# Shifting every SBUF tensor that TensorE reads to a 2048-byte boundary, with small tensors and a filler in front

## The reference, cut to what matters

```
x = conv7(x, softmax(weight))                  # 8192 tokens x 192
h = x @ w_in;  x = (h * clip(h + 3, 0, 6) / 6) @ w_out
h = x @ w_in2; y = where(h > 0, h, exp(min(h, 0)) - 1) @ w_out2
```

## Time and profile before

| | |
|---|---|
| Time, median of 3 runs | 1156.77 us (1155.81 to 1157.89) |
| The profiled execution: its time | 1156.3 us |
| The profiled execution: span from first to last instruction | 1154.5 us |
| PE busy | 1149.2 us (100% of the span), 9744 matmuls |
| PEld, weight loads | 937.8 us (81%), 9744 loads |
| DVE busy | 903.5 us (78%) |
| ACT busy | 632.5 us (55%) |
| POOL busy | 40.4 us (3%) |
| Mean granted TensorE clock | 1.000 of full speed |

### The profile page before, as it was taken

How to read it: one execution, slowest core, us unless ns; L and a number is a source line. 1 busy time by engine, 2 the same in 40 slices (tenths; PEclk the granted TensorE clock), 3 DMA queues, 4 the chain that set the end, 5 groups by cost and what they waited for, 6 DMA issues and landing times.

```text
span 1154.5 us, 24081 instructions
## 1 busy us (share of the span) xinstructions
PE 1149.2 (100%) x9744; PEld 937.8 (81%) x9744; DVE 903.5 (78%) x963; ACT 632.5 (55%) x684; POOL 40.4 (3%) x36
## 2 busy tenths in 40 slices
PE   9999999999999999999999999999999999999998
PEld 6888888888888888888888888888888888888886
DVE  7897887878778787787877878788787887876766
ACT  6665655546555555555555555555554555546544
POOL 4422000000000000000000000000000000000000
PEclk9999999999999999999999999999999999999999
DMA  4310010100101001010010100101000010000000
GB/s 151 115 38 28 1 33 0 32 0 0 32 0 32 0 0 32 0 32 0 0 32 0 32 0 0 32 0 32 0 18 14 0 32 0 9 5 10 6 2 28
DMA packets 14760, 22.48 MB, mean 19 GB/s; under 512 B 1424, under 2 KB 5520, under 8 KB 14736
## 3 DMA queue, kind: packets, MB, share of 16 engines
q1 hardware_dynamic: 14592, 22.12, 6.1%
q10 hardware_dynamic: 144, 0.01, 0.0%
HBM read 15.83 MB, written 6.29 MB: 19 GB/s over the span
## 4 chain that ended last, share of the span: by engine, by line
PE 99%; DMA 1%; ACT 0%; SPq 0%; DVE 0%; issue 0%; DVEq 0%; ACTq 0%
PE h_ps L674 39%; PE acc_a L688 23%; PE h_ps L681 21%; PE acc_b L697 15%; DMA xnext_b<-x_win 1%; PE acc_a L830 0%; PE h_ps L705 0%; PE acc_a L760 0%; DVE hidden L522 0%; PE acc_a L737 0%; ACT hidden L340 0%; PE acc_a L744 0%; PE acc_a L738 0%; PE acc_b L739 0%; PE acc_b L745 0%; PE acc_b L754 0%
## 5 line engine op out<-in xcount | busy, mean ns | idle before, releaser
L350 ACT CAST g_hi<-hidden 128x1024 fp32r<-128x1024 f32 x255 | 268.0, 1051 | 351.0 <-DVE hidden L527 237.5
L531 DVE TENSOR_TENSOR g_lo<-hidden,g_hi 128x1024 fp32r<-128x1024 f32 x255 | 313.1, 1228 | 127.6 <-ACT g_hi L350 127.6
L688 PE MATMUL acc_a<-g_hi,wout_hi_a 64*128 64x512 f32 x1012 | 398.2, 393 | 0.0
L688 PE MATMUL acc_a<-g_hi,wout_lo_a 64*128 64x512 f32 x1012 | 397.8, 393 | 0.0
L674 PE MATMUL h_ps<-in_lo_a,win_hi_a 64*128 64x512 f32 x1012 | 397.7, 393 | 0.0
L674 PE MATMUL h_ps<-in_hi_a,win_lo_a 64*128 64x512 f32 x1012 | 397.2, 392 | 0.0
L674 PE MATMUL h_ps<-in_hi_a,win_hi_a 64*128 64x512 f32 x1012 | 396.6, 392 | 0.0
L697 PE MATMUL acc_b<-g_hi,wout_b 64*128 64x512 f32 x1012 | 357.2, 393 | 0.0
L688 PE MATMUL acc_a<-g_lo,wout_hi_a 64*128 64x512 f32 x1012 | 317.4, 393 | 0.0
L697 PE MATMUL acc_b<-g_lo,wout_b 64*64 64x512 f32 x1012 | 314.9, 390 | 0.0
L522 DVE SCALAR_TENSOR_TENSOR hidden<-hidden,h_ps 128x1024 f32<-128x1024 f32 x128 | 156.2, 1221 | 77.5 <-ACT hidden L340 77.5
(11 more groups left out here) (109 smaller groups left out, 1207.7 us busy)
## 6 DMA issues: line engine op xcount, KB each, us to landing
xwin_a<-x_win SPq DMA_DIRECT2D x16, 259.0 KB, 2.7
raw_in<-w_in SPq DMA_DIRECT2D x8, 512.0 KB, 4.3
out_t<-out_a SPq DMA_DIRECT2D x16, 256.0 KB, 2.9
xwin_b<-x_win SPq DMA_DIRECT2D x15, 259.0 KB, 2.9
raw_out<-w_out SPq DMA_DIRECT2D x8, 384.0 KB, 3.6
out_t<-out_b SPq DMA_DIRECT2D x16, 128.0 KB, 2.3
xnext_b<-x_win SPq DMA_DIRECT2D x1, 259.0 KB, 6.1
taps<-tap_w ACTq DMA_DIRECT2D x1, 7.0 KB, 2.6
```

The lines of the kernel that those rows point to most:

```text
L350: nc.scalar.copy(g_hi[:, g % PARTS, :], hidden[:, g % 2, :]).then_inc(hi_ready, 1)
L531: nc.vector.tensor_tensor(g_lo[:, g % PARTS, :], hidden[:, g % 2, :], g_hi[:, g % PARTS, :].bitcast(F32), ALU.subtract).then_inc(lo_ready, 1)
L688: return nc.tensor.matmul(acc_a[acc][:, :], w[HALVES[r], g * CPG + c, :], x[HALVES[r], g % PARTS, c * TOK:(c + 1) * TOK], start=g == 0 and ...
```

## The change

The change edits only the order in which SBUF tensors are created, and adds one tensor that nothing uses. `ident`, `taps`, `tap_stat` and `three` are created first, then a `filler` of 1280 bytes a partition; `diag`, `xnext_b`, `xwin_a` and `xwin_b` are created last. On every engine the instructions and their order are the same, row for row, before and after. Only the addresses differ:

| Tensors | Bytes past a multiple of 2048, before | after |
|---|---|---|
| `win_*`, `wout_*`, `raw_in` | 128 | 0 |
| `raw_out0`, `raw_out1` | 128, 1152 | 0, 1024 |
| `conv_a`, `conv_b` | 192 | 0 |
| `in_*`, `hidden`, `g_hi`, `g_lo`, `half_b*`, `sum_b1`, `out_*` | 288 | 0 |
| `diag` | 864 | 0 |
| `xwin_a`, `xwin_b`, `xnext_b` | 128, 160, 320 | 1568, 1600, 1536 |

```
+        ident = sb("ident", [P, 2, DB])
+        taps = sb("taps", [P, 2, TAPS])
+        tap_stat = sb("tap_stat", [P, 2, 3])
+        three = sb("three", [P, 1])
+        sb("filler", [P, 320])
+
         win_hi_a = [sb(f"win_hi_a{m}", [P, FF], F32R) for m in range(2)]
...
         raw_out = [sb(f"raw_out{s}", [P, CPP, D]) for s in range(STAGES)]

-        xwin_a = sb("xwin_a", [DA, WIN])
-        xwin_b = sb("xwin_b", [2 * DB, WIN])
         conv_a = sb("conv_a", [DA, TOK])
         conv_b = sb("conv_b", [2 * DB, TOK])
-        taps = sb("taps", [P, 2, TAPS])
-        tap_stat = sb("tap_stat", [P, 2, 3])
...
-        three = sb("three", [P, 1])
+        diag = sb("diag", [P, TAPS, P])
         xnext_b = sb("xnext_b", [2 * DB, WIN])
-        ident = sb("ident", [P, 2, DB])
-        diag = sb("diag", [P, TAPS, P])
+        xwin_a = sb("xwin_a", [DA, WIN])
+        xwin_b = sb("xwin_b", [2 * DB, WIN])
```

## The result

The changed kernel takes 1131.31 us (1130.99 to 1131.97, 4 runs) against 1156.7 us (1155.81 to 1157.89, 4 runs): a ratio of 0.978, with a 95% interval of 0.976 to 0.980. It is 25 us faster. The time lies in the predicted range, but the forecast called likeliest, no change, is wrong.

A forecast was written before the change was run, and what follows sets the result against it. PE was taken to bound the kernel through the distance between its matmul starts, 233.5 ns a pair. All terms were taken as 0, so the time stays at 1156.5 us, with a range of 1123 to 1168 us (0.84).

The forecast's parts named there:

- no change: Whole kernel: the time does not depend on the addresses and stays at 1156.5 us; chance 0.68.
- What bounds the kernel: Steady stage: only the distance between matmul starts on PE, 233.5 ns a pair, can move the time by much.
- The 20 ns over 213.3 and the suspect: Steady pairs: 233.5 ns against 213.3 at one column a cycle; the reading of the moving operand is suspected.
- Moving operands: Steady pairs: starts go from 288 to 0 past a multiple of 2048; taken as 0, at most 85 us.
- Weight operands: Steady weight chunks: chunks 7 and 9 show the same steps, so taken as 0, at most 12 us back.
- a piece less for each row: Moving rows fetched in 64-byte pieces, 32 in place of 33: 6.7 ns a pair, giving 1124 us; chance 0.09.
- the whole excess goes: All 17.7 ns a steady pair come from the address, 85 us, giving 1071 us; 0.09 for more than one piece less.
- the two reads of TensorE meet: Weight loads and moving stream hinder each other after the change: 6 ns a pair, 29 us, giving 1185 us; chance 0.14.
- The Trainium skill's 16-byte lines: Moving rows: a 2048-byte row from 288 or from 0 touches 128 SBUF lines either way, so 0.
- DVE, ACT and DMAs at 0: Other engines and loads: small changes stay hidden under PE's work, so 0, with 0.6 us either way for DMAs.
- the single stream near the end stays at about 232 ns: Sign of a right prediction: four full-row matmuls near the end, 232.5 ns each before, keep their distance.

The follow-up runs named there:

- all at 32: Changed kernel with a filler 32 bytes longer, so weights and moving operands alike begin 32 bytes past a multiple of 2048: 1131.06 us, ratio 0.978.
- the first two runs: Kernel before with 32 bytes put ahead of `in_hi_a0`: 1153.85 us; changed kernel with a filler 32 bytes longer: 1131.06 us.
- short loads: Most steady matmuls use only 64 of their 128 weight columns: 1141.73 us in the kernel before, 1137.15 us in the changed one.

## Why the prediction was right in its range and wrong in its reason

- **What bounds the kernel**: right. Only the distance between pairs changed, and the time with it.
- **The 20 ns over 213.3 and the suspect**: half right. The convolution's step of 215.8 ns was read as "replacing the weights does not cost 20 ns in itself", and the suspect was the moving read alone. The convolution is no witness for the full rate: by the change its own distance goes from 224 to 0 modulo 256 at the first tap, and its step stays at 215.8 ns. At the full rate it is the moving read and the load together, by their distance, that make 5.3 of the 20 ns.
- **"Moving operands: I take 0, because the only moving start that varies in this trace changes nothing"**: this step failed. It asked for the effect of a start address by itself. That is indeed nothing (all at 32: 1131.1 us); the effect lies in the distance, 25.5 us over 4812 pairs, which the convolution did not test at the full rate.
- **"Weight operands: I take 0"**: this failed too, and for a reason worth seeing. Chunks 7 and 9 in the earlier trace rows begin at different places, but all chunks are multiples of 512 bytes apart, so their distances to the moving rows are the same modulo 256. The comparison could not have shown the effect.
- **The rival "a piece less for each row"**, which carried the lower end of the range: its 1124 us came near the result by its size only. Its mechanism is out by the first two runs. That the range from 1123 us up held the 1131.31 us is therefore luck: a bound from a mechanism that isn't there, beside a likeliest forecast of no change (0.68) that was wrong.
- **The rival "the whole excess goes"**: too large. Of the 17.7 ns a pair, 5.3 went.
- **The rival "the two reads of TensorE meet"** had the right place and the wrong sign. It took the equal start as the collision. Its price, 6 ns a pair, was close to the 5.3 ns measured, but the layout before was the one that paid.
- **The Trainium skill's 16-byte lines** ("SBUF — State Buffer", Specifications) gave 0, and starts are in fact without effect; as a forecast of this change the rule failed, and it says nothing of two readers. The measurement decides.
- **DVE, ACT and DMAs at 0**: right. The subtraction's 1228 ns and PE's waits are unchanged. `xnext_b` landed 0.8 us sooner, but the start didn't become shorter (100 matmuls by 19.3 us, 102 before).
- **The sign "the single stream near the end stays at about 232 ns"**: weak. Over the four steps that the prediction used it does stay (1118.47 to 1119.40 us, 232.5 ns); only over 18 steps does its gain of 2.7 ns show.

## What to carry to other kernels

Where TensorE reads float32r rows at the full rate with a new weight load for each matmul, look at the distance in bytes between the weights and the moving operand in a partition, modulo 256: here 0 was best and 32 or 160 cost 2%, and a pad of 96 bytes gave the whole gain. An address that varies in a trace is a test of an address effect only if it varies modulo what matters; here all that varied at the full rate was the place of the chunk, in multiples of 512. A result that lies near a rival's price is no evidence for the rival's mechanism, and one run that keeps the price and removes the mechanism (all at 32) is worth more.

## What was not expected of the hardware

The distance between two operands of TensorE changes the time of matmuls that wait for nothing: 228.2 against 233.5 ns a pair, and it repeats after 256 bytes where that was tried (0, 256 and 512 alike). Distance 64 is nearly as good as 0 (one execution), while 128 keeps only about 30% of the gain (ratio 0.993 against 0.978) and 192 about a tenth (0.998). The float32 convolution, whose windows and weights moved as well (`xnext_b` from 320 to 1536 and `diag` from 864 to 0 past a multiple of 2048), keeps its 215.8 ns. A single full-rate stream over all 128 rows gains 2.7 ns a step, half of the 5.3 of a pair. Still open: what it is in SBUF or in TensorE that repeats each 256 bytes, why 64 differs from 192, why a single stream gains half, why the short loads slow the changed kernel, and where the other 12 ns over the convolution's 215.8 go; short loads did not remove them.
